# Unread products in two of TensorE's waits, and w_in's first two pieces split in the prologue

## The reference

```python
for t in range(S):
    new_re = ar * S_re - ai * S_im
    new_im = ar * S_im + ai * S_re
    S_re, S_im = (new_re + kv, new_im)
    y[:, :, t] = np.einsum('bhd,bhde->bhe', q[:, :, t], S_re)
...
h = x @ w_in
sp = np.where(h > 20.0, h, np.log1p(np.exp(np.minimum(h, 20.0))))
out = (h * np.tanh(sp)) @ w_out
...
e_idx = np.argmax(x @ w_gate + modality_bias[modality_id], axis=1)
out[mask] = gate_w[mask, None] * (np.maximum(x[mask] @ w1[e], 0.0) @ w2[e])
```

## Time and profile before

| | us |
|---|---|
| median of 3 runs | 1014.54 |
| the profiled execution | 1014.67 |
| its span | 1012.9 |
| PE busy | 971.2 (96%) |
| PE in the chain that ended last | 90% |
| DVE busy | 714.6 (71%) |
| ACT busy | 574.0 (57%) |

### The profile page before, as it was taken

One profiled execution on the slowest core, in us unless ns is written; L12 is line 12 of the kernel. 1 busy time (PEld: TensorE's weight loads), 2 busy tenths in 40 slices (PEclk: granted clock), 3 DMA queues, 4 the chain that ended last, 5 costly groups with the idle time before them and its releaser, 6 DMA issues.

```text
span 1012.9 us, 19018 instructions
## 1 busy us (share of the span) xinstructions
PE 971.2 (96%) x6658; PEld 940.5 (93%) x6659; DVE 714.6 (71%) x1317; ACT 574.0 (57%) x1069; POOL 90.1 (9%) x148
## 2 busy tenths in 40 slices
PE   4888799999999999999999999999999999999996
PEld 3778798999999999999999999999999999999995
DVE  4656998988888888888898877888843333663332
ACT  6557886876777777778687665464122323222231
POOL 2000000000000000000000000000022222442221
PEclk9799999999999999999999999999999999999998
DMA  9702212222221221122121211003161111421110
GB/s 203 217 18 33 40 24 40 41 64 40 40 64 40 40 64 25 32 64 40 39 42 48 41 24 33 1 24 123 36 219 39 46 39 39 158 91 39 39 47 24
DMA packets 146230, 58.69 MB, mean 58 GB/s; under 512 B 131321, under 2 KB 140551, under 8 KB 146160
## 3 DMA queue, kind: packets, MB, share of 16 engines
q1 hardware_dynamic: 139056, 42.61, 17.6%
q0 software_dynamic: 3904, 10.44, 3.3%
q10 hardware_dynamic: 3200, 4.72, 1.3%
HBM read 48.21 MB, written 10.03 MB: 57 GB/s over the span
## 4 chain that ended last, share of the span: by engine, by line
PE 90%; ACT 4%; DVE 3%; issue 2%; DMA 0%; POOL 0%; SPq 0%; ACTq 0%; DVEq 0%; POOLq 0%
PE bank L1717 20%; PE bank L1698 19%; PE bank L1933 14%; PE bank L1944 11%; PE bank L1622 4%; PE bank L1661 4%; PE bank L1609 4%; PE bank L1663 3%; PE bank L1644 3%; PE bank L1556 1%; PE bank L1563 1%; PE bank L1924 1%; PE bank L1905 1%; PE bank L1687 1%; PE bank L1747 1%
## 5 line engine op out<-in xcount | busy, mean ns | idle before, releaser
L1933 PE MATMUL bank<-xg_t,w_sb 128*128 128x128 f32 x1296 | 149.2, 275 | 0.7 <-DVE xg_t L1511 0.7
L1933 PEld LDWEIGHTS bank<-xg_t,w_sb 128*128 128x128 f32 x1296 | 148.4, 192 | 1.2 <-issue 1.2
L1698 PE MATMUL bank<-x_hi,w_in_hi 128*128 128x384 f32 x384 | 141.4, 368 | 1.9 <-DVE x_lo L1112 1.9
L1717 PE MATMUL bank<-w_out_hi,g_hi 128*128 128x392 f32 x378 | 139.2, 368 | 0.0
L1698 PE MATMUL bank<-x_hi,w_in_lo 128*128 128x384 f32 x384 | 131.1, 341 | 0.0
L1698 PE MATMUL bank<-x_lo,w_in_hi 128*128 128x384 f32 x384 | 131.1, 341 | 0.0
L1717 PE MATMUL bank<-w_out_hi,g_lo 128*128 128x392 f32 x378 | 128.7, 340 | 0.0
L1717 PE MATMUL bank<-w_out_lo,g_hi 128*128 128x392 f32 x378 | 128.7, 340 | 0.0
L971 ACT ACTIVATE he<-bank 128x128 f32<-128x128 f32 x216 | 59.8, 277 | 98.4 <-PE bank L1933 96.2
L785 ACT ACTIVATE hid<-bank 128x384 f32<-128x384 f32 x128 | 62.2, 486 | 84.1 <-PE bank L1698 83.4
L975 ACT ACTIVATE o_sb<-bank,gate_now 128x384 f32<-128x384 f32 x27 | 15.7, 580 | 113.9 <-PE bank L1944 113.9
(11 more groups left out here) (316 smaller groups left out, 2071.2 us busy)
## 6 DMA issues: line engine op xcount, KB each, us to landing
w_sb<-in_moe_w_dram SPq DMA_DIRECT2D x8, 1536.0 KB, 7.9
ab<-in_a_re_dram SPq DMA_DIRECT2D x24, 192.0 KB, 2.9
ab<-in_a_im_dram SPq DMA_DIRECT2D x24, 192.0 KB, 3.2
x_rows<-x_sb ACTq DMA_DIRECT2D x8, 576.0 KB, 3.1
qk_raw<-in_q_dram SPq DMA_DIRECT2D x22, 192.0 KB, 3.4
qk_raw<-in_k_dram SPq DMA_DIRECT2D x22, 192.0 KB, 3.5
v_in<-in_v_dram SPq DMA_DIRECT2D x22, 192.0 KB, 2.8
w_out_sb<-in_moe_w_out_dram SPq DMA_DIRECT2D x4, 768.0 KB, 6.2
```

Of the source, the lines that this page charges most:

```text
L1698: last = mm(bank_h[f % 2][:, 0:TT], w[:, kk, f * P:(f + 1) * P], x[:, m % 2, kk], start=(kk == 0 and i == 0), stop=(kk == KD - 1 and i == 2))
L1717: last = mm(bank_x2[t][:, 0:DE], g[:, u % RING, f % QF, t * P:(t + 1) * P], w[:, f], start=(f == 0 and i == 0), stop=(f == FT - 1 and i == 2))
L1933: last = mm(bank_h[f % 2][:, 0:P], w1_sb[par][:, kk, f * P:(f + 1) * P], xg_t[:, kk], start=(kk == 0), stop=(kk == KD - 1))
```

## The change

`stay_awake` moves to the top of PE's program and takes the place that it writes to. It is called twice more: 13 products between chunk 0's second and third turn, and 6 products in gap 1 of block 0, behind `turn_qk(3, 0)` and ahead of `gate_step(10)`. Both write columns 256 to 383 of `bank_x2[2]`, which hold nothing at that time. On ACT `split_w_in(0)` moves up to behind `real_seed(4)`, and `split_w_in(1)` comes in behind `log_mag(4)`; on DVE `split_w_in(0)` moves to behind `slopes(4)` and `split_w_in(1)` to behind `logs(4)`. The two pieces that are left go at gaps 2 and 18, and gap 10 has none.

```diff
-    W_IN_GAPS = (0, 2, 10, 18)
+    W_IN_FIRST, W_IN_GAPS = 2, (2, 18)
...
-                        if g in W_IN_GAPS[1:]:
-                            split_w_in(W_IN_GAPS.index(g))
+                        if g in W_IN_GAPS:
+                            split_w_in(W_IN_FIRST + W_IN_GAPS.index(g))
...
             real_seed(4)
+            split_w_in(0)
             attend(1, 8)
             take_wt(7)
             log_mag(4)
+            split_w_in(1)
             scales(3)
             attend(0, 9)
             angles_next()
             turn_angle(3)
             turn_angle(4)
-            split_w_in(0)
...
             slopes(4)
+            split_w_in(0)
             mask(2, 0)
             mask(2, 1)
             take_kv(2)
             next_state(2)
             logs(4)
+            split_w_in(1)
             add_carry(3)
             attend(0, 9)
             attend(1, 9)
-            split_w_in(0)
             attend(2, 9)
...
+            def stay_awake(spare, count):
+
+                for _ in range(count):
+                    mm(spare, ident[:], earlier[:], start=True, stop=True)
...
                         attend(ch, p)
+                    if m == 0 and g == 1:
+                        stay_awake(bank_x2[2][:, 2 * P:3 * P], 6)
                     if m == 0 and g <= FT - GATE_FIRST:
                         gate_step(GATE_FIRST + g)
...
             turn_qk(0, 1)
+            stay_awake(bank_x2[2][:, 2 * P:3 * P], 13)
             turn_qk(0, 2)
...
-            stay_awake(11)
+            stay_awake(bank_h[0][:, 0:P], 11)
```

More of the change, by code:

```diff
@@ L1900, in _ @@
                 early_ranks(s_chosen, s_ranked)
-            def stay_awake(count):
-                for _ in range(count):
-                    mm(bank_h[0][:, 0:P], ident[:], earlier[:], start=True, stop=True)
             pe.wait_ge(h_copied[0], FT // 2 * NT)
-            stay_awake(11)
+            stay_awake(bank_h[0][:, 0:P], 11)
             pe.wait_ge(chosen_ready, 2)
@@ L1913, in _ @@
             mm(bank_b[:, GL * E:(GL + 1) * E], ones[:], run[:, GL], start=True, stop=True).then_inc(ranks_ready, 1)
-            stay_awake(25)
+            stay_awake(bank_h[0][:, 0:P], 25)
             for g in range(NG):
@@ L1946, in expert_tile @@
                 last.then_inc(o_ready, 1)
-            stay_awake(28)
+            stay_awake(bank_h[0][:, 0:P], 28)
             turn_tokens(0)
```

## The result

The changed kernel took a median of 1008.49 us over five runs (1007.33 to 1010.41), against 1014.54 us before. The ratio is 0.9941, 95% interval 0.9926 to 0.9955. One of five runs of the kernel before, 1221.98 us, lies far above its other four (1013.99 to 1015.93) and isn't in the ratio. The gain is 6.0 us, 0.6%; the forecast was 8.6, within a range of 1005.0 to 1009.3. The profiled execution was the slowest of the five, 1010.41 us, so what follows explains 4.3 us of gain in detail. Of the other four only the time and the mean granted clock are known: 0.994 in one, as in the profiled run, 0.996 in the median run, and 0.997 in the two of 1007.33 and 1007.88 us.

A forecast was written before the change was run, and what follows sets the result against it. PE was taken as the bound, full from about 124 us, so gains ahead of 123.18 us last. 7.0 for the first three parts plus 1.9 made 8.9, less 0.3: 8.6 us, forecast 1006.0 us, range 1005.0 to 1009.3.

The forecast's parts named there:

- Part one: 13 products before chunk 0's third turn keep the clock full from 33 to 43 us: 3.8 us gained.
- Part two: w_in's first piece split earlier, in the prologue, brings the first hidden product 1.65 us earlier.
- The exact cover on VectorE: VectorE's split of w_in's first piece fits its 1.63 us wait before 60.81 us, costing 0 to 0.1 us.
- Part three: 6 products in the 1.56 us wait before the gate step at 79.67 us hold the clock: 1.55 us gained.
- Part four: No w_in piece at gap 10, so chunk 4's products start 1.8 to 1.9 us earlier, after a 2.0 us PE wait.
- The sum: Gain of all parts at the start of chunk 4's products, 123.18 us: 7.0 + 1.9 = 8.9 us.
- the charge: 0.3 us taken off the 8.9 us gain for covers that are exact, leaving 8.6.
- its first rival: Clock falls at the new 2.0 us wait before chunk 4's products, costing about 1.5 us: 1007.5 us, chance 0.25.
- the case in which the 13 products do not hold the clock: Before chunk 0's third turn, 3.8 us becomes between -1.5 and 2.2: 1007.6 to 1011.3 us, chance 0.12.
- The fall between the second and the third hidden product: Clock falls among turns and eight-column products, about 77 to 80.5 us, costing about 1.5: 1007.5 us, chance 0.10.
- The pieces' gain at gap 10: Rival: moving the pieces gives nothing there, or VectorE's prologue piece delays the mask; 1.9 less, 1007.9 us, chance 0.08.
- Products into the same columns: Rival: unread products to one place in a bank wait for each other, 16.1 us lost: about 1027 us, chance 0.02.

The follow-up runs named there:

- the two filled kernels: Kernel before plus products in four waits (13, 6, 7 at gap 13, 8 in block 1): with w_in's first piece moved, 1007.76 us; with no piece moved, 1012.03 us.
- both waits filled: Changed kernel plus 7 unread products at gap 16 of block 0 and 8 at gap 2 of block 1: 1005.11 us, and 1005.38 us when repeated.
- 7 more products: Changed kernel plus 7 unread products at gap 16 of block 0, in the wait before the products of chunk 4: 1008.09 us.
- pieces alone: Changed kernel without the 13 and the 6 products, so only the pieces of w_in are moved: 1014.52 us, ratio 0.9996 to the kernel before.
- with transposes: Changed kernel with 26 transposes of 128x128 in place of the 13 products: 1009.23 us.
- half fillings: Kernel with 13, 6, 7 and 8 products at four places, cut to 7, 3, 4 and 4: 1007.50 us.

## Why the prediction came out as it did

**What bounds the kernel.** Right. TensorE's waits between 120 and 700 us are the same as before but for the one that changed, and whatever was won at the products of chunk 4 and not taken back by the clock was there at the end of the MLP: 6.1 us in the changed kernel.

**Part one, 3.8 us.** Measured 4.1 in the changed kernel and with the 13 products alone, 4.0 when they are taken away again. The working by PE's own repetition held; 0.3 us of the rest is that the whole sequence started that much earlier (the third turn at 35.03 instead of 35.33). The burst was 3.07 us long, 3.0 worked out, and it cost nothing.

**Part two, 1.65 us.** 5.83 us up to the first hidden product less 4.11 is 1.7; 1.86 between the two filled kernels. The exact cover on VectorE held, so the 0.3 us that I charged for covers was not needed. PE's wait for x fell to 0.52 us, a little under the 0.7 named.

**Part three, 1.55 us.** Right in its place and in its sign. What the other three parts leave of the 9.3 us is 1.6 to 1.8. Taking the 6 products away lost 2.5 us, with 6.8 us at half speed; I had sized it by the 3.4 us of one profile, and the length of a fall turned out not to be a constant (3.4, 6.8 and 10.2 us at this same place in three kernels, and none at all in a fourth).

**Part four, 1.8 to 1.9 us.** 1.7 to 1.9 by the filled kernels. So was the wait: 1.88 us, ending at 113.86, where I had 2.0 and 114.3.

**The sum** at the products of chunk 4 was 8.9 us before the charge; measured 9.3. The kernels with both waits filled, whose clock stays full and whose gather is on time, took 1005.1 and 1005.4 us, where 1014.5 less 9.3 is 1005.2. So the parts and their sum were right, with 0.3 us charged for nothing.

**The step that failed** is the choice between the forecast and its first rival. I had the new wait of 2.0 us, its place, and the two rows that spoke for and against a fall, and gave the fall 0.25. It came in both profiles of the changed kernel and in three of the four other profiles that have this wait open. The row that I let decide, 1.91 us of idleness at 70 to 72 with a full clock, was one outcome of something that has two: 2.1 us before a turn of chunk 6 dropped the clock in the profiles of two kernels (7 more products, pieces alone) and not in seven others, and 1.56 us before the gate step held it in one. A row in which nothing happened shows that it need not happen, not that it won't. Its price was too low as well: 1.5 us, taken from a low stretch of 3.4 us, when the stretch was 6.8 us and cost 3.2. In five other profiles a fall of 3.4 us behind the third mark did cost about what I had put on it, 1.6 us (590.9 us to the end of the MLP instead of 589.3), so it is the length that I had wrong.

**The second miss** is a cost that stands in no rival: PE's wait for the experts' gather, 1.4 to 1.5 us. It was in both profiles of the changed kernel, in those with 7 more products, with transposes and with half fillings, and not in that of before nor in the other eight. I treated all that lies behind 124 us as carried along, which is true of TensorE's own work but not of the experts' transfers. What decides it is open. The kernels with both waits filled have the same spacing of load and scatter and do not have the wait; the one with half fillings ends its MLP within 0.2 us of them and has it.

**Luck.** The median of 1008.49 lies within the range, but not for the reasons that the range was drawn for. It reaches to 1009.3 for the case in which the 13 products do not hold the clock, and they held it. What used that room was a fall of the clock about twice as dear as the rival's, and a gather that I had not named; the two profiled executions with both, 1010.41 and 1011.67 us, lie outside. How the other ten runs divide between the two costs isn't shown. By an estimate from the profiles, a fall of 6.8 us would lower a run's mean clock by 0.0034 (6.8 x 0.5 / 1007), so the four runs at 0.997, the figure of the filled kernel, can't have had one; yet they took 1007.3 to 1008.0 us, 2 to 3 more than the filled kernel's 1005.1, and a gather of 1.4 us covers only a part of that.

**The other rivals.** The 13 products did hold the clock. The fall between the second and the third hidden product did not come in any profile with the 6 products. The pieces' gain at gap 10 did arrive. Products into the same columns did not wait for each other, 26 in 3.07 us. The pieces alone, which the prediction never priced without the products, gained nothing in the median.

## What to carry to other kernels

List every wait of TensorE above about one microsecond after a change, not only those that the change fills: work taken off another engine makes TensorE arrive earlier and wait in a new place, and here that wait cost 3.2 of the 9.3 us won. Unread products in such waits cost nothing here, where they ended 0.1 to 0.35 us before the release. Filling the four waits that had dropped the clock turned 1008.5 and 1009.3 us, with spreads of 3 and 4 us, into 1005.1 and 1005.4 us, with spreads of 0.6 and 2.0. Of that, up to 3.2 us is the clock; 1.4 is a gather that came in time, and that the filling brought this about isn't shown. Put the products into the wait that is the last one left: with 7 of them three gaps earlier, 2.4 us stayed open before the products of chunk 4 and the clock fell all the same. Price a fall of the clock by the longest low stretch that any profile shows, and settle part prices by the start times of one instruction in kernels whose clocks are full, not by medians.

## What the runs showed of the hardware

The same wait, in front of the same work, may or may not drop TensorE's clock: 2.07 us before the turn of chunk 6 did at 160.78 in the kernel with 7 more products, and 2.06 us did not at 170.3 in the kernel before; 1.88 to 1.90 us before the products of chunk 4 did in five profiles (3.4 or 6.8 us at half speed) and did not in a sixth; 1.56 us before the gate step did in three kernels (3.4, 6.8 and 10.2 us at half speed) and did not in a fourth. Low stretches ahead of the tail measured 3.4, 6.8 or 10.2 us in all fourteen profiles, and nothing between. Behind the third mark one of 3.4 us cost 1.4 to 1.6 us up to the end of the MLP and one of 6.8 cost 3.2.

26 fp32 transposes of 128x128 in 3.00 us held a full clock just as 26 instructions of products in 3.07 us.

At the end of every profile the clock is low for the last 5.0 to 7.6 us, well after the last product; nothing runs on TensorE there, so the mean granted clock of a run (0.997) is below 1 even where no product was slowed.
